# An expert layer behind attention: the expert to go first is chosen on the chip, its weights are split during the attention, and its first slot runs beside the last batch's routing

## The reference

```python
a = softmax(causal(q @ k.T / 8)) @ v                      # B=4, H=8, S=576, D=64
mem = (phi(q) @ M_prev) / (phi(q) @ z_prev + 1e-6)         # phi(x) = elu(x) + 1
x = (g * mem + (1 - g) * a).transpose(0, 2, 1, 3).reshape(2304, 512)   # g = sigmoid(beta)

e_idx = argmax(x @ w_gate, axis=1)                         # one of 8 experts per token
for e in range(8):
    m = e_idx == e
    y[m] = gate_w[m] * sigmoid(x @ w_output_gate)[m, e] * (relu(x[m] @ w1[e]) @ w2[e])
h = y @ w_in                                               # 512 -> 2048
out = (h - tanh(h)) @ w_out
```

## Time and profile before

| | us |
|---|---|
| median of 3 runs | 1036.23 (1035.51 to 1036.79) |
| the profiled execution | 1038.67 |
| its span, first to last instruction | 1036.8 |
| busy: PE / DVE / ACT / POOL | 975.0 / 645.9 / 503.6 / 473.5 |

### The profile page before, as it was taken

The page is one execution under the profiler, slowest core; times in us unless marked ns, Lnnn a source line. Parts: engine busy times, 40 slices in busy tenths (PEclk is TensorE's granted clock), DMA queues, the critical chain, the costliest instruction groups (busy, mean ns, idle before and its releaser), DMA issues.

```text
span 1036.8 us, 16594 instructions
## 1 busy us (share of the span) xinstructions
PE 975.0 (94%) x5377; PEld 812.5 (78%) x5378; DVE 645.9 (62%) x1241; ACT 503.6 (49%) x1045; POOL 473.5 (46%) x334
## 2 busy tenths in 40 slices
PE   3999999899729999999999999999999999999998
PEld 2667667576527888888888878899999999999997
DVE  3687686867634444444444438777777777777764
ACT  5777677686242211022112036556565555555554
POOL 5565586675489733047636136432232322322221
PEclk9999999999859999999999999999999999999999
DMA  9465566531385533146473201010010010100001
GB/s 209 119 167 158 158 189 173 145 106 39 137 319 198 188 122 121 51 143 220 173 272 132 71 31 42 1 31 32 1 61 1 9 53 1 31 31 1 32 1 31
DMA packets 51008, 103.64 MB, mean 100 GB/s; under 512 B 7424, under 2 KB 16640, under 8 KB 50432
## 3 DMA queue, kind: packets, MB, share of 16 engines
q1 hardware_dynamic: 34416, 56.68, 18.8%
q10 hardware_dynamic: 13616, 36.70, 9.7%
q0 software_dynamic: 2912, 9.44, 2.9%
HBM read 82.62 MB, written 20.19 MB: 99 GB/s over the span
## 4 chain that ended last, share of the span: by engine, by line
PE 84%; DVE 10%; POOL 2%; issue 2%; ACT 1%; DMA 1%; ACTq 0%; SPq 0%; DVEq 0%
PE scores L1427 6%; PE scores L1429 6%; PE scores L1428 6%; PE average L1383 4%; PE average L1382 4%; PE average L1384 4%; PE average L1261 4%; PE scores L1371 4%; PE scores L1369 4%; PE scores L1370 4%; POOL ring L535 2%; PE scores L1165 2%; PE average L1444 2%; PE mix L1445 2%; PE turned L1444 2%; PE average L1445 2%
## 5 line engine op out<-in xcount | busy, mean ns | idle before, releaser
L572 POOL TENSOR_TENSOR g_lo<-g,g_hi 128x384 fp32r<-128x384 f32 x96 | 97.8, 1019 | 275.4 <-ACT g_hi L775 274.9
L535 POOL TENSOR_TENSOR ring<-ring 128x2048 fp32r<-128x2048 f32 x30 | 137.2, 4603 | 109.6 <-ACT ring L715 105.8
L715 ACT ACTIVATE ring<-ring 128x2048 fp32r<-128x2048 f32 x30 | 55.7, 1906 | 183.5 <-PE scores L1371 81.7
L1427 PE MATMUL scores<-yt_hi,w_in_hi 128*128 128x384 f32 x384 | 131.1, 341 | 1.7 <-DVE yt_lo L1128 1.7
L1429 PE MATMUL scores<-yt_hi,w_in_lo 128*128 128x384 f32 x384 | 129.5, 337 | 0.0
L1428 PE MATMUL scores<-yt_lo,w_in_hi 128*128 128x384 f32 x384 | 129.2, 336 | 0.0
L765 ACT ACTIVATE sq<-scores 128x384 f32<-128x384 f32 x96 | 47.2, 491 | 164.3 <-PE scores L1429 164.3
L1120 DVE COPY_PREDICATED ser<-big,th 128x384 f32<-128x384 int32 x96 | 118.9, 1239 | 3.3
L1115 DVE TENSOR_TENSOR ser<-ser,sq 128x384 f32<-128x384 f32 x96 | 55.8, 582 | 96.4 <-ACT ser L768 96.4
L598 ACT ACTIVATE prob<-scores,nmx 128x128 f32<-128x128 f32 (+3 forms) x128 | 66.3, 524 | 46.3 <-DVE nmx L850 45.9
L1369 PE MATMUL scores<-ring,xt_hi 128*128 x200 | 81.1, 406 | 3.1 <-DVE xt_lo L1064 1.7
(11 more groups left out here) (251 smaller groups left out, 2480.9 us busy)
## 6 DMA issues: line engine op xcount, KB each, us to landing
ring<-in_w ACTq DMA_DIRECT2D x13, 2048.0 KB, 9.0
q_sb<-in_qt SPq DMA_DIRECT2D x48, 288.0 KB, 4.4
k_sb<-in_kt SPq DMA_DIRECT2D x32, 288.0 KB, 4.3
xin<-x_sorted SPq DMA_DIRECT2D x27, 256.0 KB, 2.7
y_sorted<-y_sb SPq DMA_DIRECT2D x25, 256.0 KB, 2.1
v_sb<-in_v SPq DMA_DIRECT2D x16, 256.0 KB, 2.8
ring<-in_w SPq DMA_DIRECT2D x8, 512.0 KB, 4.8
w_out_sb<-in_w_out ACTq DMA_DIRECT2D x1, 4096.0 KB, 15.9
```

The lines of the kernel that those rows point to most:

```text
L535: pool.tensor_tensor(ring[:, ring_at(k), 1, part], ring[:, ring_at(k), 1, part].bitcast(F32), ring[:, ring_at(k), 0, part].bitcast(F32), A ...
L572: pool.tensor_tensor(g_lo[:, t % GRING, :], g32[:, t % 2, :], g_hi[:, t % GRING, :].bitcast(F32), ALU.subtract).then_inc(g_lo_ok, 1)
L1427: mm(ff_h(t), w_h, yt_hi[:, j % 2, c, :], start=c == 0, stop=False)
```

## The change

A DVE function chooses, after batches 0 and 1 are counted, the expert with the most tokens (`largest`) and makes the order: the chosen expert takes place 0, expert 0 takes the chosen one's place, the others stay (`order`, in round 12). All loads of expert weights read the expert's number from that order. SP loads w1 and w2 of the chosen expert at the end of its rounds 13 and 14; ACT and POOL split both in rounds 14 to 16, in sixteenths, the last four low parts after the attention. The first slot's tokens (the first 128 rows of the chosen expert, all of batches 0 and 1) are loaded after the last scores. PE turns them among the last logits and begins the first `up` behind the count. DVE's table code is cut in two and the first slot's ReLU and split stand between its parts. The first slot's `down` comes before the second's `up`. ACT issues the loads of units 3 and 4 only when the second slot's tokens have landed. `swap` puts the counts and row bases in the new order. Slots 1 to 6 are written out and the loop runs over the other 18.

```diff
+HIGH = {(14, 0): (0,), (14, 1): (1,), (14, 2): (2,), (14, 3): (3,), (15, 0): (4, 5), (15, 1): (6, 7), (15, 2): (8,), (15, 3): (9,),
+        (15, 4): (10,), (16, 0): (11, 12), (16, 1): (13, 14), (16, 2): (15,)}
+LOW_AHEAD = {14: (0,), 15: (3, 4, 5, 6, 7, 8), 16: (9, 10, 11)}
+LOW_BEHIND = {14: (1, 2)}
...
-                if 3 <= n < 3 + 2 * CD:
-                    load_first_expert(n - 3)
-
+                if n in (13, 14):
+                    if n == 13:
+                        sp.wait_ge(r_order, 1)
+                    first = sp.value_load(order_i[0:1, 0:1], min_val=0, max_val=E - 1)
+                    for c in range(CD):
+                        load_first_expert((n - 13) * CD + c, first)
+
+            row = sp.value_load(first_i[0:1, 0:1], min_val=0, max_val=E * REG)
+            sp.wait_ge(q_split, NP)
+            sp.wait_ge(scored, NP * QT)
+            sp.dma_start(xin[:, 0, :], xs[bass.ds(row, P), :]).then_inc(xin_ok[0], 16)
...
-                if n == NP:
-                    for i in range(2, QT):
-                        scatter(B - 2, i)
+                for q in LOW_BEHIND.get(n, ()):
+                    early_low(q)
...
+            for i in range(2, QT):
+                scatter(B - 2, i)
             for i in range(QT):
                 scatter(B - 1, i)
+            pool.wait_ge(r_slots, 1)
+            for q in range(12, SIXTEENTHS):
+                early_low(q)
             pool.wait_ge(r_tails, 1)
-            for k in range(1, UNITS):
+            for k in range(2, UNITS):
...
+                r, part = ring_at(q // 8), slice(q % 8 * EIGHTH, (q % 8 + 1) * EIGHTH)
+                act.wait_ge(w_ok[r], landed(q // 8))
+                if q == 8:
+                    act.wait_ge(k_split, NP)
+                    act.wait_ge(q_split, NP)
+                act.activation(ring[:, r, 0, part], ring[:, r, 1, part].bitcast(F32), ACT.Copy).then_inc(early_hi, 1)
...
-                    if i == 3 and EARLY <= n < EARLY + 8:
-                        early_high(n - EARLY)
+                    for q in HIGH.get((n, i), ()):
+                        early_high(q)
...
-            for k in range(1, 3):
-                convert(k)
+            convert(2)
             act.wait_ge(scattered, 16 * TILES)
-            load_unit(act, 3)
-            load_unit(act, 4)
+            act.wait_ge(xin_ok[1], 16)
+            load_unit(act, 3, expert_of(act, 3))
+            load_unit(act, 4, expert_of(act, 4))
...
+            def order():
+
+                rs(dve.tensor_scalar(chosen[:, :], desc[:, :], first_s[:, 1:2], None, ALU.is_equal))
+                rs(dve.tensor_tensor(order_f[:, :], chosen[:, :], expert_f[:, :], ALU.mult))
+                rs(dve.tensor_tensor(order_f[:, :], expert_f[:, :], order_f[:, :], ALU.subtract))
+                rs(dve.tensor_scalar(order_f[:, 0:1], first_s[:, 1:2], -1.0, float(E), ALU.mult, ALU.add))
+                dve.tensor_scalar(first_i[:, :], order_f[:, 0:1], float(REG), None, ALU.mult)
+                dve.tensor_scalar(base_o[:, :], order_f[:, :], float(REG), None, ALU.mult)
+                dve.tensor_copy(order_i[:, :], order_f[:, :]).then_inc(r_order, 1)
...
+            relu(0)
+            dve.tensor_copy(step_e[:, 0:1], gap_o[:, 0:1])
...
-            rs(dve.tensor_tensor(table[:, 2, :], row0, spare, ALU.subtract))
+            dve.tensor_tensor(table[:, 2, :], row0, spare, ALU.subtract).then_inc(r_slots, 1)
+            split_hid(0)
...
+            first_up()
             turn_hid(0)
...
+            first_down()
+            pe.wait_ge(r_table, 1)
+            up(1)
+            turn_in(0, 2, t_ps[0])
+            turn_hid(1)
```

More of the change, by code:

```diff
@@ L403, in store_y @@
                 sp.dma_start(ys[bass.ds(t * P, P), :], y_sb[:, k % 2, :]).then_inc(y_out[k % 2], 16)
-            for k in range(XIN):
+            for k in range(1, XIN):
                 load_x(k, k)
@@ L970, in _ @@
                     if 0 <= b < B - 1 and i == 2 and half == 3:
-                        place_rows(b, m_ps, RANKS)
+                        place_rows(b, m_ps, LOGITS if b == CHOICE else RANKS)
+                    if b == CHOICE + 1 and half == 0 and i == 2:
+                        largest()
+                    if b == CHOICE + 1 and half == 0 and i == 4:
+                        order()
                     if i == 0 and n >= 2:
@@ new lines, in _ @@
+            gates_of(0, B - 1)
+            split_x(0, o_ps[1])
+            take_logits(B - 1, t_ps[1], 0)
+            pick(B - 1)
+            place_rows(B - 1, t_ps[0], 0)
+            rows_of(B - 1)
+            dve.tensor_copy(base_n[:, :], t_ps[0][:, QT * E:(QT + 1) * E])
+            rs(dve.tensor_copy(fill_i[:, :], t_ps[0][:, QT * E:(QT + 1) * E]))
+            dve.sem_inc(r_fill, 1)
+            n_e, slots_e, end_e, start_e, gap_o, n_o, part_e, step_e = (small_e[:, r, :] for r in range(8))
@@ new lines, in _ @@
+            dve.wait_ge(r_exp, 4)
+            gates_of(B - 1, B)
+            wide = [P, TILES, E]
+            swap(n_e, gap_o)
+            rs(dve.tensor_tensor(hot2[:, :, :], hot[:, 1:TILES + 1, :], n_e[:, None, :].to_broadcast(wide), ALU.mult))
+            rs(dve.tensor_reduce(row_f[:, 1, :], hot2[:, :, :], AX.X, ALU.add))
+            rs(dve.tensor_tensor(y_u[:, :], row_f[:, 0, :], row_f[:, 1, :], ALU.subtract))
+            for b in range(0, B, 2):
+                a, z = b * QT + QT - 1, (b + 1) * QT + QT - 1
+                dve.tensor_copy(y_u[D:P, a:a + 1], y_u[0:D, z:z + 1])
+                last = dve.tensor_copy(gate[D:P, a:a + 1], gate[0:D, z:z + 1])
@@ new lines, in _, with slot @@
+            rs(last)
+            dve.sem_inc(r_tails, 1)
+            def slot(t, at, half):
+                relu(t)
+                split_x(t + 1, t_ps[0])
+                copy_y(t - 1, half, at - 1)
+                split_hid(t)
+            split_x(1, t_ps[0])
+            copy_y(0, 0, 0)
+            relu(1)
+            split_x(2, t_ps[0])
+            split_hid(1)
+            for t in range(2, PEELED):
+                slot(t, t, (t - 1) // 2)
+            with dve.Fori(0, (SLOTS - PEELED) // SPAN) as i:
+                for at in range(PEELED, PEELED + SPAN):
+                    slot(i * SPAN + at, at, i * (SPAN // 2) + (at - 1) // 2)
@@ L1345, in _, with turn_in @@
                         turn_x(b * QT + 4, s_ps[m % 2][1])
+            def turn_in(round, k, bank):
+                pe.wait_ge(xin_ok[k % XIN], round * 16 + 16)
+                for c in range(CD):
+                    last = pe.transpose(bank[:, c * P:(c + 1) * P], xin[:, k % XIN, c * P:(c + 1) * P], ident[:, :])
+                last.then_inc(x_turned, 1)
             for i in range(QT):
@@ L1392, in turn_hid, with slot @@
                     last.then_inc(h_turned, 1)
[L1394 to L1405 removed]
+            def slot(t, at, round):
+                pe.wait_ge(relu_done, t * 2)
+                up(t)
+                turn_in(round, at + 1, t_ps[0])
+                down(t - 1)
+                turn_hid(t)
+            first_up()
+            turn_hid(0)
+            first_down()
[3 more added lines that the diff above has]
+            turn_hid(1)
+            for t in range(2, PEELED):
+                slot(t, t, (t + 1) // XIN)
+            with pe.Fori(0, (SLOTS - PEELED) // SPAN) as i:
+                for at in range(PEELED, PEELED + SPAN):
+                    slot(i * SPAN + at, at, i * (SPAN // XIN) + (at + 1) // XIN)
             down(SLOTS - 1)
```

216 lines of the change are left out of this document (112 added, 104 removed).

## The result

The changed kernel takes 1045.16 us in the median of 4 runs (1045.02 to 1047.16), against 1036.24 of the kernel before: ratio 1.0087, 95% interval 1.0070 to 1.0103. It is slower by 9 us, where 8.5 were forecast. The profiled execution of it has a span of 1043.2 us. I read it in the order of the parts of the prediction.

A forecast was written before the change was run, and what follows sets the result against it. Bound by TensorE's hole at 282 to 302 us, weight arrival in rounds 14 and 15, and expert order. -14.5 + 8.7 + 3 + 1 + 10.3 = +8.5 us on 1036.2: 1044.7, said as 1044.5; range 1033 to 1051.

The forecast's parts named there:

- Part 1: Head of the experts: slot 0 runs beside the routing, filling TensorE's hole; gains 14.5 us.
- Part 2: Attention round 14: ACT's split waits for w1, delaying k_hi and the scores of pair 15; costs 8.7 us.
- Part 3: Attention round 15: ACT waits for w2 the same way, other splits cost nothing; costs 3 us.
- Part 4: Choosing the expert: twelve small DVE instructions, seven of them in round 12; costs 1 us.
- Part 5: New expert order: two one-slot experts together, PE idles 7.8 us before slot 18, restarts 2.4 us slower; costs 10.3 us.
- the absorbed waits: Rival, attention: w1 and w2 land before PE, DVE and POOL run out of work; 1033.7 us, chance 12%.
- the absent late wait: Rival, expert stage: PE's wait at slot 18 does not arise; 1034.4 us, chance 12%.
- the three cases that were named for faster: Attention waits absorbed (12%), half of no slot 18 wait (12%), neither wait (6%, about 1023 us); faster given 0.20.

The follow-up runs named there:

- loads_ahead: Changed kernel with SP issuing the chosen expert's w1 and w2 loads before its wait for v's buffer in rounds 13 and 14: 1036.55 us, ratio 0.9991.
- both: Changed kernel with the loads_ahead edit, and the experts ahead of the chosen one moved back one place instead of a swap: 1026.3 us, ratio 0.9889.

## Why the prediction was right

**Part 1, the head:** forecast 14.5 us won, of which 0.5 had been taken off for the transposes ahead of the count; behind the count that is 15.0, and 15.0 are measured. Behind the count the hidden tile was to be ready after 14.0 us, and the first `down` began after 13.9; the third `up` was to come after 31.2, and came after 31.3. Two small errors of opposite sign are in it, so that the last digit is luck: two table instructions were held up by POOL for 1.1 us each, so that PE waited 1.18 us for the second tile's low part (first `down` to second `up` 9.4 us, not 8.6), and the second slot with its bubble took 8.0 us, not 8.6.

**Part 2, the wait in round 14:** forecast 8.7, measured 8.8. The sum has two errors that cancel. SP issued the four pieces from 238.67 on, 1 us later than I took (the read of the index took 1.3 us, not 0.6), and they had landed by 246.73, 8.1 us after the first issue, where I took 9.0 from the row of a whole 2 MB load. The 6.8 us of the Trainium skill (DMA: Bandwidth & Descriptors) would have let ACT go on at 245.5 (the page fits it for DMAs that POOL's queue issues, and these go on SP's); for the second group, which SP issued from 263.09 on and ACT could use at 272.37, 9.3 us later, it is further off. The trace does not agree with the page's figure here. The path is as forecast: POOL's q split of pair 15 ran at 252.65, 10.8 us later than in before (11.1 forecast).

**Part 3, the wait in round 15:** forecast 3, and the count ended at 295.19, where the parts say 282.4 + 8.7 + 3 + 1 = 295.1. From the last load of v to the end of the count the changed kernel takes 35.1 us and before 30.9, which is 3.7 more without the 0.5 of the transposes. The second half of this part was wrong, though the time did not show it: POOL's low parts were to cost nothing, and at most 1 us by late adds. In `loads_ahead` and `both`, where the two waits no longer cover them, 3 us of delay stay in round 14, and not by late adds. 0.9 to 1.6 of them went when the parts no longer held up DVE's small instructions; the other 1.5 go with a lower clock of TensorE, whose cause is open. With the waits gone these 3 us come to light, which fits that undoing the waits gave back 9.9 us and not 11.7.

**Part 4, choosing:** forecast 1 us, and the number came out in part by luck. By the loads of v, rounds up to 12 ran 1 us ahead of before (217.32 against 218.36) and round 13's came 0.3 behind (235.16 against 234.82): round 13 is 1.4 us longer. But the seven instructions of `order` stand in round 12 (214.22 to 215.82), and 1.05 us of round 13's 1.4 are in one DVE instruction that the sum did not have. First before, then the changed kernel:

```profile
218.13 0.17 DVE L876 SCALAR_TENSOR_TENSOR wts<-sums,inv_l 128x10 f32<-128x10 f32 x1
218.04 1.22 DVE L912 SCALAR_TENSOR_TENSOR wts<-sums,inv_l 128x10 f32<-128x10 f32 x1
```

POOL runs beside it in both, but not at the same moments, and the row does not end where one of POOL's does, so what held it is not shown. No run takes the choosing out.

**Part 5, the order:** forecast 7.8 us of idle time and 2.4 of restart. The idle time is 7.7 us, released by POOL, with the clock at 0.50 behind it. The restart was dearer in the sum than in the trace: that `up` took 7.5 us (531.09 to 538.60) and not 8.0, 1.9 more than one at the full clock. Undoing the order gave back 10.9 us by ratio and 9.0 by span, and 10.2 to 10.4 by the distance from the third `up` to the end.

**The sum:** +8.5 forecast, +8.9 by the medians. The spans differ by 6.4 only, because the profiled execution of before was itself 2.4 us above the median, as the prediction said. Of the rivals, neither the absorbed waits nor the absent late wait is borne out; each of the two has its own experiment in which it is taken away. One slip is in the chances: the three cases that were named for faster add up to 0.24, not to 0.20.

## What to carry to other kernels

A split that waits for a load, put into an engine's list ahead of work that others need, costs what the load is late, and the load is late by what its own queue waits for before it: look at the queue's wait ahead of the issue first (here one swap of two lines in SP's program was worth 9.9 us). Where weights stream through a ring, write out for each load after whose last use it may start: two short experts next to each other give it too little time, and in the other order tried here TensorE waited for none. And an idle stretch of POOL is free only if DVE does not need the same access to SBUF: before a POOL instruction is moved there, read what DVE runs beside it.

## What the runs showed of the hardware

POOL holds DVE up, for whole instructions. A POOL `tensor_tensor` on SBUF (1.27 us for 128x512) makes a DVE instruction that has two SBUF inputs, or a small fp32 cast or `tensor_scalar` on SBUF, last until POOL is through: 0.20 us became 1.31, 0.17 became 1.27, 0.75 became 1.87. Twice DVE did not get in between three such instructions of POOL either: 0.37 us became 4.31, and 0.35 became 4.02, beside 3.75 and 3.71 us of POOL. In other places it did get in after each one (the rows of the head after the change, and those of round 14 in `both`); what decides that stays open. Nor does every long row end with one of POOL's: the one of 1.22 us in round 13 does not. `TENSOR_REDUCE` and instructions that read PSUM were not slowed in the same stretches (0.19, and 0.42 for the mixing). The Trainium skill (SBUF — State Buffer, "SBUF: two separate sides") says that the port pair that the two share is an exclusive lock for a whole instruction, taken by a DVE instruction in a two-port mode, or by one with two SBUF inputs against a POOL instruction that reads SBUF. The traces agree, with the rows above.
